# Rounding the high parts of two mixtures' weights on ScalarE and Pool in place of casting DMAs

## The reference

```python
def _moe_ref(x, w_gate, w1, w2):
    logits = x @ w_gate            # 3072 x 8, then pairs in falling order,
    ...                            # each token once, at most N // E = 384 per expert
    for e in range(E):
        mask = assigned == e
        h = np.maximum(x[mask] @ w1[e], 0.0)      # w1[e]: 320 x 1024
        out[mask] = h @ w2[e]                     # w2[e]: 1024 x 320
...
def _moe2_ref(x, expert_emb, tau, w1, w2):
    logits = xn @ en.T / tau       # xn, en: rows of unit length
    expert_idx = np.argmax(logits, axis=1)
    ...
    for e in range(E):
        mask = expert_idx == e
        h = np.maximum(x[mask] @ w1[e], 0.0)
        out[mask] = gate_w[mask, None] * (h @ w2[e])
```

## Time and profile before

| | |
|---|---|
| time, median of 3 executions | 1084.75 us (1078.61 to 1091.55) |
| the profiled execution: span from the first to the last instruction | 1103.3 us |
| PE busy / DVE busy / Pool busy / ACT busy in that span | 816.0 / 567.8 / 392.8 / 217.4 us |
| mean granted TensorE clock | 0.828 |
| bytes moved by the DMAs that Pool issues | 58.16 MB of 137.26 |

### The profile page before, as it was taken

How to read it: one execution, slowest core, us unless ns; L and a number is a source line. 1 busy time by engine, 2 the same in 40 slices (tenths; PEclk the granted TensorE clock), 3 DMA queues, 4 the chain that set the end, 5 groups by cost and what they waited for, 6 DMA issues and landing times.

```text
span 1103.3 us, 18868 instructions
## 1 busy us (share of the span) xinstructions
PE 816.0 (74%) x5803; PEld 679.3 (62%) x5804; DVE 567.8 (51%) x1558; ACT 217.4 (20%) x451; POOL 392.8 (36%) x334
## 2 busy tenths in 40 slices
PE   2989888982233333039999999994799999998496
PEld 1777777861222222028888888874577888776385
DVE  7877778357766677302656566648222222222121
ACT  3221222000000000002332322331222222221121
POOL 4443334035200000533554465546034254356411
PEclk9998899695555555559999888996899999999699
DMA  4444443264300000233766576555454755653200
GB/s 133 136 142 119 130 119 107 68 196 127 122 0 0 0 0 0 78 109 83 247 193 189 185 236 197 150 175 172 132 174 125 215 171 167 191 156 118 89 27 1
DMA packets 70227, 137.26 MB, mean 124 GB/s; under 512 B 14791, under 2 KB 53968, under 8 KB 66098
## 3 DMA queue, kind: packets, MB, share of 16 engines
q1 hardware_dynamic: 43282, 67.16, 20.8%
q0 software_dynamic: 11008, 58.16, 16.2%
q10 hardware_dynamic: 15904, 11.53, 4.0%
HBM read 77.36 MB, written 14.48 MB: 83 GB/s over the span
## 4 chain that ended last, share of the span: by engine, by line
PE 53%; DVE 17%; issue 9%; another core or an unknown queue 1%; ACT 1%; DVEq 0%; POOL 0%; ACTq 0%; POOLq 0%
PE bank L1304 8%; PE bank L1305 7%; PE bank L1306 7%; PE bank L1290 4%; PE bank L1327 3%; PE bank L1425 2%; PE bank L1443 2%; PE bank L1332 2%; PE bank L1328 2%; PE bank L1329 2%; PE bank L1259 2%; PE bank L1361 2%; DVE routing_arena L859 2%; DVE routing_arena L892 2%; DVE routing_arena L954 1%
## 5 line engine op out<-in xcount | busy, mean ns | idle before, releaser
L1304 PE MATMUL bank<-w_hi,hT_hi 128*128 (+1 forms) x440 | 148.3, 337 | 19.1 <-issue 16.5
L1306 PE MATMUL bank<-w_hi,hT_lo 128*128 (+1 forms) x440 | 142.7, 324 | 1.8 <-issue 1.8
L1305 PE MATMUL bank<-w_lo,hT_hi 128*128 (+1 forms) x440 | 143.3, 326 | 1.0 <-issue 1.0
L1290 PE MATMUL bank<-routing_arena 128*8 128x16 bf16 x1344 | 43.3, 173 | 103.7 <-DVE routing_arena L859 103.7
L652 POOL TENSOR_TENSOR w_lo<-w_raw,w_hi 128x2560 fp32r<-128x2560 f32 x16 | 91.0, 5685 | 76.1 <-DMA w_hi<-w_raw 75.6
L606 POOL DMA_INDIRECT x_sorted<-tokens,routing_arena x48 | 47.3, 986 | 187.7 <-DVE routing_arena L942 161.6
L1290 PEld LDWEIGHTS bank<-routing_arena 128*8 128x8 bf16 x1344 | 37.5, 93 | 108.8 <-DVE routing_arena L859 108.8
L1304 PEld LDWEIGHTS bank<-w_hi,hT_hi 128*128 128x128 f32 x440 | 89.5, 203 | 21.9 <-issue 21.7
L634 POOL TENSOR_TENSOR w_lo<-w_raw,w_hi 128x2048 fp32r<-128x2048 f32 x16 | 73.0, 4564 | 69.0 <-DMA w_hi<-w_raw 68.1
L1305 PEld LDWEIGHTS bank<-w_lo,hT_hi 128*128 128x128 f32 x440 | 89.5, 203 | 1.8 <-issue 1.8
L1306 PEld LDWEIGHTS bank<-w_hi,hT_lo 128*128 128x128 f32 x440 | 89.1, 202 | 1.4 <-issue 1.4
(11 more groups left out here) (250 smaller groups left out, 1806.7 us busy)
## 6 DMA issues: line engine op xcount, KB each, us to landing
w_raw<-in_moe_w SPq DMA_DIRECT2D x16, 1280.0 KB, 6.7
w_hi<-w_raw POOLq DMA_DIRECT2D x16, 1280.0 KB
w_raw<-in_moe_w SPq DMA_DIRECT2D x16, 1024.0 KB
w_hi<-w_raw POOLq DMA_DIRECT2D x16, 1024.0 KB, 4.7
w_hi<-w_raw POOLq DMA_DIRECT2D x32, 256.0 KB, 5.8
mlstm_arena<-in_q SPq DMA_DIRECT2D x64, 120.0 KB
routing_arena<-x_sorted ACTq DMA_DIRECT2D x31, 160.0 KB
w_raw<-in_moe_w SPq DMA_DIRECT2D x16, 256.0 KB
```

The lines of the kernel that those rows point to most:

```text
L1290: last = T.matmul(bank[6][0:E, 0:WAYS], choice[:, :, g], cmp_b[:, g, :], start=(g == 0), stop=(g == G - 1))
L1304: T.matmul(dst, a_hi, b_hi, start=first, stop=False)
L1305: T.matmul(dst, a_hi, b_lo, start=False, stop=False)
L1306: return T.matmul(dst, a_lo, b_hi, start=False, stop=last)
```

## The change

Pool's casting DMAs go. For sets 0, 1 and 10 to 15 Pool rounds with a copy of its own, 128 x 3072 for w1 and 128 x 2560 for w2. For sets 2 to 8 (w1: 2 to 9) ScalarE rounds, in the middle of its step of stage one: three copies of 128 x 1024 for set e + 2 and, from step 1 on, two of 128 x 1280 for the w2 of set e + 1. Pool rounds the w2 of set 9. Pool's order in stage one becomes low w1 of set n, low w2 of set n - 1, scatters. SP loads the last 64 rows of w1 twice, once for each half of the partitions (256 KB more per set). DVE's tables get one more instruction: the number of blocks of each expert is at least 1.

```diff
--- before.py
+++ after.py
@@ -357,7 +357,8 @@
                 if n:
                     sp.wait_ge(w1_ready, 2 * n)
                 sp.dma_start(w1_raw[:, 0:2, :], a[e, 0:256, :].rearrange("(k p) f -> p k f", p=128)).then_inc(raw1_ready, 16)
-                sp.dma_start(w1_raw[64:128, 2, :], a[e, 256:DM, :]).then_inc(raw1_ready, 16)
+                for h in range(2):
+                    sp.dma_start(w1_raw[64 * h:64 * h + LOW, 2, :], a[e, 256:DM, :]).then_inc(raw1_ready, 16)
                 if n:
                     sp.wait_ge(w2_ready, n)
                 sp.dma_start(w2_raw[:, :, :], b[e, :, :].rearrange("(k p) d -> p k d", p=128)).then_inc(raw2_ready, 16)
@@ -445,6 +446,19 @@
                     act.wait_ge(h3_ready, FT * e + f + 1)
                     nc.scalar.activation(hT_hi[:, f, :], bank[f % 2][:, 0:BPE * 128], ACT.Relu).then_inc(hh3_ready, 1)
 
+            def w1_hi3(n, s):
+
+                act.wait_ge(raw1_ready, 48 * (n + 1))
+                for k in range(KT):
+                    nc.scalar.activation(w1_hi[:, s, k, :], w1_raw[:, k, :], ACT.Copy).then_inc(hi1_ready, 1)
+
+            def w2_hi3(n, s):
+
+                act.wait_ge(raw2_ready, 16 * (n + 1))
+                for h in range(2):
+                    k = slice(h * FT // 2, (h + 1) * FT // 2)
+                    nc.scalar.activation(w2_hi[:, s, k, :], w2_raw[:, k, :], ACT.Copy).then_inc(hi2_ready, 1)
+
             def next_rows3(e):
                 act.wait_ge(ids3_ready, e)
                 load_rows3(e)
@@ -469,6 +483,9 @@
                     x_hi3(e + 1)
                 if not isinstance(e, int) or e < E - 2:
                     next_rows3(e + 2)
+                w1_hi3(e + RING, p)
+                if not isinstance(e, int) or e:
+                    w2_hi3(e + 1, 1 - p)
                 if not isinstance(e, int) or e:
                     squares3(e - 1, 1 - p)
                     exps3(e - 1)
@@ -606,55 +623,49 @@
                 pool.indirect_dma_start(dst, bass.IndirectOffsetOnAxis(ap=dest[:, g:g + 1], axis=0),
                                         tokens[:, slot, :], None).then_inc(scattered, 16)
 
-            def scatter3(r, n):
-
-                pool.wait_ge(w1_ready, 2 * n + 2)
+            def scatter3(r):
+
                 pool.wait_ge(route3_done, r + 1 + 1)
                 for b in range(BPE):
                     scatter(x_sorted2, BPE * r + b, G + BPE * (r % 2) + b)
 
-            def load_hi1(n):
+            def make_hi1(n):
 
                 s, m = n % RING, n - RING
-                pool.wait_ge(raw1_ready, 32 * (n + 1))
-
-                if 0 <= m < E:
-                    pool.wait_ge(h3_ready, FT * (m + 1))
-                elif m >= E:
+                pool.wait_ge(raw1_ready, 48 * (n + 1))
+                if m >= E:
                     pool.wait_ge(slot1_free, m - E + 1)
-                pool.dma_start(w1_hi[:, s, 0:2, :], w1_raw[:, 0:2, :]).then_inc(hi1_ready, 16)
-                for h in range(2):
-                    pool.dma_start(w1_hi[64 * h:64 * h + LOW, s, 2, :], w1_raw[64:64 + LOW, 2, :]).then_inc(hi1_ready, 16)
+                nc.gpsimd.tensor_copy(w1_hi[:, s, :, :], w1_raw[:, :, :]).then_inc(hi1_ready, KT)
 
             def make_lo1(n):
                 s = n % RING
-                pool.wait_ge(hi1_ready, 48 * (n + 1))
-                if n:
-                    pool.wait_ge(w2_ready, n)
+                pool.wait_ge(hi1_ready, KT * (n + 1))
                 nc.gpsimd.tensor_tensor(w1_lo[:, s, :, :], w1_raw[:, 0:2, :], w1_hi[:, s, 0:2, :], ALU.subtract).then_inc(w1_ready, 1)
                 pool.wait_ge(w1_ready, 2 * n + 1)
+                if n >= RING:
+                    pool.wait_ge(scattered, 16 * (G + BPE * min(max(n - RING - 1, 0), E)))
                 nc.gpsimd.tensor_tensor(w1_hi[64:128, s, 2, :], w1_raw[64:128, 2, :], w1_hi[64:128, s, 2, :], ALU.subtract).then_inc(w1_ready, 1)
-
-            def load_hi2(n):
+                pool.wait_ge(w1_ready, 2 * n + 2)
+
+            def make_hi2(n):
+
                 s, m = n % RING, n - RING
                 pool.wait_ge(raw2_ready, 16 * (n + 1))
-
-                if 0 <= m < E:
-                    pool.wait_ge(yb_ready, 1 + BPE * (m + 1))
+                if m == E - 1:
+                    pool.wait_ge(yb_ready, 1 + BPE * E)
                 elif m >= E:
                     pool.wait_ge(slot2_free, m - E + 1)
-                pool.dma_start(w2_hi[:, s, :, :], w2_raw[:, :, :]).then_inc(hi2_ready, 16)
+                nc.gpsimd.tensor_copy(w2_hi[:, s, :, :], w2_raw[:, :, :]).then_inc(hi2_ready, 2)
 
             def make_lo2(n):
                 s = n % RING
-                pool.wait_ge(w1_ready, 2 * n + 2)
-                pool.wait_ge(hi2_ready, 16 * (n + 1))
+                pool.wait_ge(hi2_ready, 2 * (n + 1))
                 nc.gpsimd.tensor_tensor(w2_lo[:, s, :, :], w2_raw[:, :, :], w2_hi[:, s, :, :], ALU.subtract).then_inc(w2_ready, 1)
 
             def split_weights(n):
-                load_hi1(n)
+                make_hi1(n)
                 make_lo1(n)
-                load_hi2(n)
+                make_hi2(n)
                 make_lo2(n)
 
             pool.wait_ge(y_done, NP + 2)
@@ -664,16 +675,13 @@
             for g in range(G):
                 scatter(x_sorted, g, g)
             for n in range(RING, E + RING):
-                load_hi1(n)
+                make_lo1(n)
                 if n > RING:
                     make_lo2(n - 1)
-                make_lo1(n)
-                load_hi2(n)
-                if n > RING:
-                    scatter3(n - RING - 1, n)
-            scatter3(E - 1, E + RING - 1)
+                    scatter3(n - RING - 1)
+            scatter3(E - 1)
+            make_hi2(E + RING - 1)
             make_lo2(E + RING - 1)
-            pool.wait_ge(tab_ready, 1)
             for n in range(E + RING, 2 * E):
                 split_weights(n)
             for b in range(NB2):
@@ -1110,6 +1118,7 @@
 
             link(V.tensor_tensor(work[:, :, :], by_expert(rem[:, :]), g128[:, :, :], ALU.is_gt))
             link(V.tensor_reduce(nblk[:, :], work[:, :, :], AX.X, ALU.add))
+            link(V.tensor_scalar(nblk[:, :], nblk[:, :], 1.0, None, ALU.max))
             link(V.memset(full[:, :], 1.0))
             link(V.tensor_tensor_scan(cumb[:, :], full[:, :], nblk[:, :], 0.0, ALU.mult, ALU.add))
 
```

## The result

The changed kernel takes 1116.61 us (median of four executions, 1110.94 to 1128.74) where the kernel before takes 1081.68: ratio 1.0292, 95% interval 1.0229 to 1.0354, slower. Measured once more, as *after_again*, the ratio is 1.0302 (1.0229 to 1.0375). One execution of the four that lies apart, 1128.74, is left out of the ratio.

The account below looks back on a forecast made before the run. PE was taken to set the end after the routing. Stage one 21.4, clock 10, routing -5 and start of stage two 2 summed to +28 us: 1113 from the median 1084.75, range 1086 to 1128.

Parts of the forecast that it names:

- Which row ends the hold: Stage one, worked step: Pool's L663 holds DVE's choices until 652.2; transposes to ranks take 22.4 us in place of 19.45.
- the first two terms of the sum: Stage one: 4 x 3.0 us for the steps of experts 3 to 6, 2 x 4.2 for experts 1 and 2.
- The sixth step: Stage one: counted among the four steps of experts 3 to 6, +3.0 us by the late choices.
- The seventh step: Last step of stage one: ScalarE rounds 3.2 us earlier without next rows or DMAs, so only +1.0 us.
- The rule of the hold: DVE and Pool: during a Pool subtraction no DVE instruction reading and writing SBUF runs; one slips in between two subtractions.
- PE's wait: Stage one, at the ranks: PE stands 3.0 us, or more if block 2 ends earlier, for the late choices.
- Clock: Stage one, after PE's standstill: half clock at the next first layer, 1.7 us in 6 steps, 10 us, range 0 to 21.
- Routing: Routing: fewer held DVE instructions gain 6 us, with slow rounding a loss of 8; taken as -5 us.
- Whether a rounding copy holds DVE: Pool's rounding copies: assumed to hold DVE; if not, routing loses some 4 us less, stage two's start 2 less.
- Start of stage two: DVE's table for stage two: two Pool instructions follow the scatters, one DVE instruction passes between; +2 us, range 0 to 3.
- Stage two: Stage two: Pool's time per set falls, but PE is busy 292 of 333 us; counted as 0.
- Rival 1: Stage one: PE's cover holds, choices at 652.0 not 655.0, only gains left; 1070, up to 1080 us; chance 0.13.

Follow-up runs that it names:

- before_again: The kernel before, unchanged, measured and traced a second time: 1082.83 us, span 1081.0 us.
- e8: e1 with SP's order turned in stage one, raw w1 of set n+1 loaded ahead of raw w2 of set n: 1071.14 us, 0.9901 of before.
- e9: e8 with set 1 split behind stage one's 24 opening scatters and Pool waiting for stage two's table before rounding set 9: 1062.40 us, 0.9797 of before.
- e10: e8 with Pool waiting for the table of stage two's blocks before it rounds set 9: 1069.13 us, 0.9853 of before.
- e5: The changed kernel with 32 unused transposes on PE ahead of the ranks in steps 1 to 6: 1107.96 us, 1.0242 of before.
- e2_again: e2 measured again, on chip C: 1080.63 us, 0.9935 of before.
- e1: The changed kernel with Pool's long w2 subtraction put behind the three scatters in steps 1 to 6: 1124.18 us, 1.0167 of before.
- e2: The kernel before with Pool rounding only sets 0, 1, 10 to 15 and last w1 rows loaded twice; casting DMAs stay in stage one: 1099.31 us, 0.9919.

## Why the prediction was right

It was +28 us (1113, range 1086 to 1128), measured was a ratio of 1.0292, which on its 1081.68 is +32, and between the two undisturbed traces +29.4. By its steps:

- **Which row ends the hold.** The worked step is met to 0.1 us: squares 9.1 us behind the transposes (9.3 before), L663 14.0 us behind them (13.9 worked out), the choices at 22.4 (22.4). Steps 1 to 6 take 22.8, 22.5, 22.5, 22.5, 22.3 and 20.7 us from transposes to ranks, before_again 19.0, 18.2, 19.4, 19.5, 19.5 and 18.0: +19.8, where the first two terms of the sum gave 20.4. The seventh step adds 0.8 (worked out 1.0).
- **The sixth step** gets its +2.7 us by another path than the one worked out, which is luck. ScalarE has no DMAs for next rows to issue there, so it rounds at once, and Pool's first subtraction starts 4.8 us behind the transposes in place of 6.9. It holds a copy that stands ahead of the logits:

```profile
731.51 4.63 POOL L643 TENSOR_TENSOR w_lo<-w_raw,w_hi 128x2048 fp32r<-128x2048 f32 x1 [19.73 <-ACT w_hi L453]
...
731.96 4.21 DVE L973 COPY tokens<-routing_arena 128x3 f32<-128x3 f32 x1 [2.54 <-PE bank L1315]
```

  PE waits 1.9 us for the logits (0.7 before), the clock is then at 0.50 for 6.8 us (3.4 before), and when PE comes to the ranks the choices are there: it does not wait for them. e8, e9 and e10 have the same 20.7 us. The prediction had seen the missing DMAs for the last step alone.
- **The rule of the hold** was taken too wide ("a DVE instruction that reads and writes SBUF does not run"). Twelve copies of one number from SBUF to SBUF (L1070) lie inside a subtraction or copy of Pool in stage two of after and take their usual 0.14 us. The prediction had that exception for stage two, and it touches no term of the sum.
- **PE's wait** was given as 3 us in six steps; it is 5.1 to 6.8 in steps 1 to 5 and nothing in the sixth. The shift is the same: in before PE ran part of block 2 at half clock, in after it runs it at full clock and then waits longer. The prediction had named this without counting it.
- **Clock.** 10 us, by half of its upper bound. The five first layers take 86.5 us against 71.8, +14.7; in after_again +16.8. Mis-sized by 5 us, inside its range. This term varies between executions of one kernel, as after_again shows. In e5, with the standstill filled, 11 of the 17 us are gone (one execution each), so most of it comes with the standstill.
- **Routing.** -5; the two traces give -3.6, after_again with before_again -2.1, after with the first trace of before -6.9. The four operations of DVE that are held while Pool splits sets 0 and 1 take 12.6 us together, in before_again 16.5, so 4 us are gained there (6 worked out). The rounding takes 2.75 and 2.33 us, taken as 2.7 and 2.2; the slow end of the bounds is out. By the Trainium skill (GPSIMD Engine Reference, "Elementwise — side-by-side cycle accounting") the first would be 2.64 us, an estimate from its 1.03 cycles per element, and the trace agrees within 5%.
- **Whether a rounding copy holds DVE**, which no row before told: it does. In the tables of stage two of after, L1132 ends 0.07 us behind Pool's copy L658, and L1133 0.04 us behind the subtraction:

```profile
795.57 2.33 POOL L658 CAST w_hi<-w_raw 128x2560 fp32r<-128x2560 f32 x1
797.99 5.57 POOL L663 TENSOR_TENSOR w_lo<-w_raw,w_hi 128x2560 fp32r<-128x2560 f32 x1
...
795.22 2.75 DVE L1132 TENSOR_TENSOR routing_arena<-routing_arena 128x31 f32<-128x31 f32 x1
798.00 5.60 DVE L1133 TENSOR_SCALAR routing_arena<-routing_arena 128x31 f32<-128x31 f32 x1
```

  The profile lets L1132 begin 0.35 us ahead of the copy, but it is held as long in after_again (2.75 us) and e8 (2.74), and in e10, where Pool's copy waits for the tables, the same operation takes 0.19 us. By the Trainium skill (SBUF — State Buffer, "Who interferes with whom") a DVE instruction with two inputs in SBUF contends with any Pool instruction that reads SBUF; the trace agrees, with these 2.75 us behind a copy of Pool.
- **Start of stage two.** +2 worked out, +2.8 measured.
- **Stage two.** 0 worked out, -8.1 measured. This step failed: I looked at PE's share and at the largest waits and put the others aside. While the casting DMAs of sets 10 to 15 ran, PE waited about 1 us at each of six blocks, 6.3 us in all, once for weights that came late; e2_again, with Pool's own rounding there, has none of these waits.
- **The standstill of before** was taken to be no part of the timed executions. before_again bears that out: it has none and takes 1082.83 us.

The term that was put too low (clock, by 5) and the one that was put too high (stage two, by 8) offset each other in part, so the sum is closer than its parts, and that is luck. The measured terms make 26.4 of the 29.4 us; no term stood for the ranks behind the last step (+1.4) or the end of the span (+0.8), and 0.8 lies between the legs. Rival 1 needed the choices 3 us earlier; e8 shows that version, and its gain of 12 us lies in the 5 to 15 of the rival. But its parts are others: in the traces 7.0 us by the opening of stage one, 2.7 in the five steps and 7.5 from the first block on, which the rival had put at nothing, less 2.8 at the start of stage two.

## What to carry to other kernels

An engine at 36% of the span can still set the time, if its long operations hold the short dependent operations of another engine whose result the bound engine waits for: look up, for each instruction of such a chain, what the other engine runs at that moment, and put the long operations where the chain is idle. When a producer is moved, follow every queue that waits for it, the loads in an in-order queue above all: e1 moved the cost into SP's stream, and only both moves together gave the gain. Shortening the blocks did not help this chain, moving them did, and a standstill of a few us is to be priced with the low clock behind it.

## What the runs showed of the hardware

**A stretch of 20 us late in stage two belongs to the execution or chip, not to the kernel.** The first trace of before and the four traces from chip A have it, at the time when Pool issues the output scatters that have piled up, 1.29 us apart; the nine others have the same burst and no such stretch. The kernel before and e2 each have one trace with it and one without. In the first trace of before one block takes 31.4 us in place of 9.16 there. The windows view of it, of before:

```profile
1016.00:1048.00 32.00, 13.93 (x54) 11.11 (x52) 4.55 (x9) 4.46 (x8) 16.50 (x17) 0.68 0.28 97
```

and of before_again:

```profile
1016.00:1048.00 32.00, 32.00 (x186) 26.87 (x185) 9.07 (x23) 8.92 (x18) 17.57 (x18) 1.00 0.32 108
```

Pool goes on at the same pace, PE does 54 matmuls in place of 186. On chip A the kernel before takes 1108.88 us, 22 to 26 us more than on chips C and B, about the length of this stretch. Its cause I can't tell.

**The granted clock falls in a step though PE is busy.** Over the five steps it is at 0.50 for 27 us in before_again, in pieces of 3.4 to 6.8 us, one in each step; where it is 6.8, PE needs 19.4 us from transposes to ranks, where it is 3.4, 18.0 to 18.2. In e8, with the same matmuls and no casting DMAs there, it is at 0.50 for 17 us and steps 2 to 5 need 17.0 to 17.2. But e2_again, with casting DMAs, has 17 us as well, so the DMAs alone don't decide it. What does wasn't tried.
